# One bucket product of the attention pair loop, issued one slot earlier (slots 3 and 9 for 4 and 10)

## The chip, the cores and the metric

The kernel runs on one core of one Trainium2 chip. The metric is the device time of one execution, in microseconds (us); lower is better. Five engines of the core matter here, each with its own queue that it works through in order: TensorE (PE) for matmuls, VectorE (DVE), ScalarE (ACT) and GpSimd (POOL) for elementwise work, and SyncE (SP), which issues transfers.

## The reference

Three stages in a row. The change lies in the first, an attention over 2 x 8 heads of 768 rows and 64 features, in which a query sees only the keys that fall into its own hash bucket (six sign bits of a projection):

```python
q_bits = (np.einsum('bhsd,dk->bhsk', q, proj) > 0).astype(np.int64)
k_bits = (np.einsum('bhsd,dk->bhsk', k, proj) > 0).astype(np.int64)
q_bucket = np.sum(q_bits * powers, axis=-1)
k_bucket = np.sum(k_bits * powers, axis=-1)
mask = q_bucket[:, :, :, None] == k_bucket[:, :, None, :]
scores = scale * np.matmul(q, k.transpose(0, 1, 3, 2))
scores = np.where(mask, scores, -1000000000.0)
attn = softmax(scores)          # written out in the reference
return np.matmul(attn, v)
```

Behind it come a two-dimensional Fourier transform with normalisation and a feed-forward block (512 to 2048 to 512), and then a gated convolution with two more products.

## The kernel before, in words

The attention works on pairs of heads, eight pairs, numbered 0 to 7 (pairs 0, 1 and 7 are written out, pairs 2 to 6 are a loop; a ninth, shortened pass ends it). A pair has twelve **slots**, 0 to 11: slots 0 to 5 make the six score tiles of its head 0 (128 queries by 768 keys each), slots 6 to 11 those of its head 1. The halves 0 to 5 and 6 to 11 are called first and second half here.

In slot s TensorE makes, in this order: the scores of tile s (L1390, four matmuls into one of two score tiles in banks 0 to 3); the transposes of the probabilities of tile s-2 (L1457), three in a part called P0 and three in P1; what PREPARE lists for the slot; in slots 3 and 9 the transposes of a finished output (use "O", L1465); and in slots 2, 5, 8 and 11 twelve matmuls of probabilities times values (L1407), at the slot's end.

PREPARE is the preparation of the next head's mask. "B" projects queries and keys to bits (L1343, then VectorE's threshold L1027). "C0" and "C1" are the **bucket products**: one matmul (L1349) of the bits with a code table for the first or the second 384 columns, after which VectorE writes two comparisons, into q_b (L1031) and k_b (L1032). Those rows of q_b and k_b enter the scores of the next head, whose first tile is six slots or less away.

On the other engines a slot is: VectorE takes the row minimum of the scores (L1039), copies P1 out (L350; in slot 9 ScalarE does that, `P1_BY_ACT`), then does the comparisons of C0 or C1, or writes the output for "O" (L1056). ScalarE copies P0 out (L350) and then takes the exponential of tile s (L727). TensorE waits for the exponential of tile s-2 before the scores of tile s.

**The scratch banks.** P0, P1, B, C0, C1 and O all go to three PSUM banks (`scratch`, numbers 0 to 2), which are dealt out in turn in program order:

```python
for s in range(SLOTS):
    uses += [(s, "P0"), (s, "P1")]
    uses += [(s, task) for task in PREPARE.get(s, [])]
    if s in OUT_SLOT:
        uses.append((s, "O"))
banks = [n % 3 for n in range(len(uses))]
```

TensorE waits before each use until the use before it in the same bank has been read out (semaphores `scratch_free0` to `scratch_free2`; `wait_free`). For a bucket product the bank is free when the second comparison, k_b L1032, is done. So each use waits for the one three places ahead of it in the list (where a pair leaves a use out, as pair 0 does with O, its place is skipped, and the banks of the others stay).

Of the kernel before, what the change touches and what calls it, by code (L numbers as in the profile page):

```python
# [6 lines left out]
def attention_fft_ffn_gate_kernel(nc, qT, kT, v, proj, w_ch1, w_ch2, w_val, conv_wT, w_out,  # L7
# [20 lines left out]
    B, H, D, S = qT.shape  # L28
# [18 lines left out]
    C0 = 512  # L47
    C1 = S - C0
# [3 lines left out]
    with ctx:  # L52
# [187 lines left out]

        PREPARE = {0: ["B"], 2: ["C0"], 4: ["C1"], 6: ["B"], 8: ["C0"], 10: ["C1"]}
        C1_SLOTS = [s for s in sorted(PREPARE) if "C1" in PREPARE[s]]
        OUT_SLOT = {3: 0, 9: 1}

# [4 lines left out]
# [4 lines that stand above are left out]
# [43 lines left out]
        def wait_drained(eng, i, use):  # L298

            need(eng, scratch_free[bank_of(i, use)], use_number(i, use))  # L300
# [29 lines left out]
        def prepared(i, s, task):  # L330

            if s >= 6:
                return i, (next(x for x in range(6) if task in PREPARE.get(x, [])), task)
            if isinstance(i, int) and i == 0:
                return -1, (0, task)
            return i - 1, (next(x for x in range(6, SLOTS) if task in PREPARE.get(x, [])), task)

# [998 lines left out]
        def _(pe):  # L1336
# [10 lines left out]
            def buckets(i, use):  # L1347

                return pe.matmul(scratch(i, use), codes[:, int(use[1][1]), :], bits_sb[:, :], start=True, stop=True)  # L1349
# [5 lines left out]
            def prepare(i, use):  # L1355
# [9 lines left out]
                else:  # L1365
                    if use[1] == "C0":

                        of_head = range(6) if use[0] < 6 else range(6, SLOTS)
                        wait_drained(pe, i, (0 if isinstance(i, int) and i < 0 else
                                             next(x for x in of_head if "B" in PREPARE.get(x, [])), "B"))  # L1370
                    op = buckets(i, use)
# [430 lines left out]
```

## Time and profile before

| | before |
|---|---|
| median of 3 runs | 630.85 us (629.72 to 631.02) |
| profiled execution, its own time | 629.69 us |
| its span in the profile | 628.0 us |
| TensorE busy | 616.9 us, 98% of the span |
| VectorE, ScalarE, GpSimd busy | 55%, 51%, 40% |
| attention, pairs 0 to 7 | from 12.8 us to some 239 us of the span |

The span is the stretch between the first and the last instruction that the profiler shows; 1.7 us of the execution's own time lie around it. Busy times are averages over stages, and TensorE's ends are modelled, so that the rows below are read for their starts and for their waits.

### The profile page before, as it was taken

How to read it: one execution, taken by the hardware profiler on the slowest of the kernel's cores; microseconds unless marked ns; L12 is line 12 of the kernel's file. 1: busy time of each engine (PE TensorE's matmuls, PEld its weight loads, DVE VectorE, ACT ScalarE, POOL GpSimd, SP SyncE). 2: the span in 40 equal slices, each digit the busy share in tenths (PEclk: the TensorE clock that was granted, in tenths of full speed). 3: DMA queues.
4: the chain of work that ended last, by engine and by line, in shares of the span. 5: the costliest groups of instructions: out<-in, count | busy, mean ns of one | idle time of the engine just before them, and what ended most of it. 6: DMA issues, size and time to landing. Idle time of an engine off the chain costs nothing.

```text
span 628.0 us, 11034 instructions
## 1 busy us (share of the span) xinstructions
PE 616.9 (98%) x3754; PEld 502.4 (80%) x3754; DVE 345.9 (55%) x587; ACT 318.0 (51%) x611; POOL 250.7 (40%) x213
## 2 busy tenths in 40 slices
PE   6899999999999999999999999999999999999998
PEld 3677776777776776988888888888888888888887
DVE  3978888788888785796211111117333333339920
ACT  4877787778787783464322222225233332444242
POOL 4544433334338664356233323327444334304140
PEclk9999999999999999999999999999999999999999
DMA  6942323323332020001211222620322211000202
GB/s 142 235 112 63 89 67 85 89 75 90 96 96 70 13 64 1 1 1 34 68 60 41 68 67 67 201 68 11 90 67 67 67 57 51 10 1 1 85 18 100
DMA packets 34411, 42.15 MB, mean 67 GB/s; under 512 B 3536, under 2 KB 22480, under 8 KB 34384
## 3 DMA queue, kind: packets, MB, share of 16 engines
q1 hardware_dynamic: 32416, 37.38, 20.7%
q0 software_dynamic: 1728, 4.02, 2.7%
q10 hardware_dynamic: 240, 0.39, 0.3%
q8 instruction: 17, 0.28, 0.2%
q14 instruction: 10, 0.08, 0.0%
HBM read 38.63 MB, written 3.15 MB: 67 GB/s over the span
## 4 chain that ended last, share of the span: by engine, by line
PE 94%; DVE 2%; ACT 1%; DMA 1%; POOL 1%; issue 1%; ACTq 0%; POOLq 0%
PE banks L1608 21%; PE banks L1594 21%; PE banks L1390 12%; PE banks L1407 11%; PE banks L1457 10%; PE banks L1671 5%; PE banks L1687 5%; PE banks L1430 2%; PE banks L1540 2%; PE banks L1343 2%; PE banks L1465 1%; DMA k_raw<-in_k 1%; PE banks L1349 1%; PE banks L1514 1%; DVE row_min L1039 1%
## 5 line engine op out<-in xcount | busy, mean ns | idle before, releaser
L1170 DVE SCALAR_TENSOR_TENSOR h_lo<-banks,h_hi 128x512 fp32r<-128x512 f32 x64 | 35.3, 557 | 169.1 <-ACT h_hi L840 169.1
L1039 DVE TENSOR_REDUCE row_min<-banks 128x1 f32<-128x768 f32 x96 | 91.8, 956 | 32.2 <-PE banks L1390 31.5
L727 ACT ACTIVATE prob<-banks,row_min 128x768 f32<-128x768 f32 x96 | 87.0, 906 | 29.6 <-DVE row_min L1039 29.5
L1594 PE MATMUL banks<-unT_hi,w_hi 128*128 128x512 f32 (+1 forms) x256 | 86.2, 337 | 0.4 <-DVE h_lo L1170 0.2
L1594 PE MATMUL banks<-unT_hi,w_lo 128*128 128x512 f32 (+1 forms) x256 | 86.2, 337 | 0.0
L1594 PE MATMUL banks<-unT_lo,w_hi 128*128 128x512 f32 (+1 forms) x256 | 86.1, 336 | 0.0
L1457 PE MATMUL banks<-ident,prob 128*128 128x128 f32 x576 | 79.3, 273 | 1.4 <-ACT probT L350 1.4
L569 POOL TENSOR_TENSOR w_lo<-w_stage,w_hi 128x512 fp32r<-128x512 f32 x32 | 45.3, 1415 | 86.2 <-ACT w_hi L758 86.2
L1457 PEld LDWEIGHTS banks<-ident,prob 128*128 128x128 f32 x576 | 68.1, 140 | 6.7 <-issue 1.9
L840 ACT ACTIVATE h_hi<-banks 128x512 fp32r<-128x512 f32 x64 | 31.2, 490 | 79.0 <-PE banks L1594 79.0
L574 POOL TENSOR_TENSOR w_lo<-w_stage,w_hi 128x512 fp32r<-128x512 f32 x32 | 42.2, 1317 | 67.3 <-ACT w_hi L763 67.3
L1407 PE MATMUL banks<-probT,v_in 128*64 128x384 f32 x384 | 69.0, 494 | 0.0
L1608 PE MATMUL banks<-h_hi,w_hi 128*128 128x512 f32 (+1 forms) x256 | 66.1, 340 | 0.0
L1608 PE MATMUL banks<-h_hi,w_lo 128*128 128x512 f32 (+1 forms) x256 | 66.0, 339 | 0.0
L1608 PE MATMUL banks<-h_lo,w_hi 128*128 128x512 f32 (+1 forms) x256 | 65.6, 338 | 0.0
L763 ACT CAST w_hi<-w_stage 128x512 fp32r<-128x512 f32 x32 | 19.9, 620 | 88.8 <-PE banks L1608 88.8
L1257 DVE SCALAR_TENSOR_TENSOR x_then_u_then_gate<-x2T,taps,x_then_u_then_gate 128x384 f32<-128x384 f32 (+1 forms) x64 | 59.0, 927 | 4.9 <-DVE x_then_u_then_gate L1257 2.6
L350 ACT COPY probT<-banks 128x384 f32<-128x384 f32 x104 | 49.0, 479 | 22.5 <-PE banks L1457 22.2
L1390 PE MATMUL banks<-k_a,q_a 128*128 128x384 f32 x192 | 57.2, 378 | 2.6 <-POOL q_a L508 1.8
L503 POOL TENSOR_TENSOR k_b<-k_raw,k_a 64x768 fp32r<-64x768 f32 x16 | 29.3, 1829 | 70.2 <-ACT k_a L710 70.1
L1390 PEld LDWEIGHTS banks<-k_a,q_a 128*128 128x128 f32 x192 | 29.6, 189 | 31.4 <-issue 28.5
L1594 PEld LDWEIGHTS banks<-unT_hi,w_hi 128*128 128x128 f32 x256 | 48.0, 188 | 7.7 <-DVE h_lo L1170 0.4
(164 smaller groups left out, 1191.0 us busy)
## 6 DMA issues: line engine op xcount, KB each, us to landing
w_stage<-in_moe_w_ch SPq DMA_DIRECT2D x64, 256.0 KB, 2.8
q_raw<-in_q SPq DMA_DIRECT2D x32, 192.0 KB, 3.3
k_raw<-in_k SPq DMA_DIRECT2D x30, 192.0 KB, 3.6
v_in<-in_v SPq DMA_DIRECT2D x16, 192.0 KB, 2.8
out<-y_out SPq DMA_DIRECT2D x11, 256.0 KB, 2.0
seq_tables_sb<-in_dft POOLq DMA_DIRECT2D x6, 386.0 KB, 3.7
wvo_stage<-in_moe_w_val SPq DMA_DIRECT2D x1, 1024.0 KB, 5.7
wvo_stage<-in_moe_w_out SPq DMA_DIRECT2D x1, 1024.0 KB, 8.5
```

The lines of the kernel that those rows point to most:

```text
L350: copy(dst, src).then_inc(scratch_free[bank_of(i, use)], 1)
L569: pool.tensor_tensor(w1_lo[:, slot, :, :], w1_stage[:, slot, :, :], w1_hi[:, slot, :, :].bitcast(F32), ALU.subtract).then_inc(w1_lo_done, 1)
L574: pool.tensor_tensor(w2_lo[:, slot, :], w2_stage[:, slot, :], w2_hi[:, slot, :].bitcast(F32), ALU.subtract).then_inc(w2_lo_done, 1)
L727: act.activation(prob[s % 2][:, :, :], s_tile(s), ACT.Exp, bias=row_min[:, s:s + 1], scale=-1.0, accum_out=row_sum[:, s:s + 1]).then_inc(e ...
L1039: dve.tensor_reduce(row_min[:, s:s + 1], s_tile(s), AX.XY, ALU.min).then_inc(min_ready, 1)
L1170: dve.scalar_tensor_tensor(out=h_lo[:, slot, at:at + size], in0=h_bank[c], scalar=0.0, in1=h_hi[:, slot, at:at + size].bitcast(F32), op0=A ...
L1257: dve.scalar_tensor_tensor(out=dst, in0=src, scalar=weight, in1=dst, op0=ALU.mult, op1=ALU.add).then_inc(conv_step, 1)
L1390: op = pe.matmul(s_tile(s)[:, c, :], lhs[:, rows], rhs[:, c * HALF:(c + 1) * HALF], start=start, stop=not start)
L1407: op = pe.matmul(PS[g * D:(g + 1) * D, 7, 0:HALF], v_in[:, h, kt, :], probT[h][:, kt, g * HALF:(g + 1) * HALF], start=(kt == 0), stop=(kt ...
L1457: op = pe.transpose(bank[:, j * P:(j + 1) * P], prob[tile % 2][:, c, j * P:(j + 1) * P], ident[:, :])
L1594: op = pe.matmul(h_bank[c], w_[:, slot, kb, :], x_[:, kb, at:at + size], start=(kb == 0 and m == 0), stop=(kb == KB - 1 and m == 2))
L1608: op = pe.matmul(acc(d, c), w_[:, slot, cols], h_[:, slot, at:at + size], start=False, stop=last, skip_group_check=True)
```

## The change

The second bucket product of each head's preparation, "C1", is listed in slots 3 and 9 in place of 4 and 10. C0 and B stay where they are, and so do the outputs in slots 3 and 9. The whole diff:

```diff
-        PREPARE = {0: ["B"], 2: ["C0"], 4: ["C1"], 6: ["B"], 8: ["C0"], 10: ["C1"]}
+        PREPARE = {0: ["B"], 2: ["C0"], 3: ["C1"], 6: ["B"], 8: ["C0"], 9: ["C1"]}
         C1_SLOTS = [s for s in sorted(PREPARE) if "C1" in PREPARE[s]]
         OUT_SLOT = {3: 0, 9: 1}
```

What it moves is seen best on TensorE in slots 3 to 5 of pair 1, here before. L1465 is O, L1349 is C1, L1457 with the first wait in a slot is P0 and with the second P1; slot 3's scores stand ahead of these rows.

```order
L1457 MATMUL banks<-ident,prob1 128x128 [waits scratch_free2,exp_done]
L1457 MATMUL banks<-ident,prob1 128x128 x2
L1457 MATMUL banks<-ident,prob1 128x128 [waits scratch_free0]
L1457 MATMUL banks<-ident,prob1 128x128 x2
L1465 MATMUL banks<-ident,outT 128x128 [waits scratch_free1,outT_copied]
...
L1457 MATMUL banks<-ident,prob0 128x128 [waits scratch_free2,exp_done]
L1457 MATMUL banks<-ident,prob0 128x128 x2
L1457 MATMUL banks<-ident,prob0 128x128 [waits scratch_free0]
L1457 MATMUL banks<-ident,prob0 128x128 x2
L1349 MATMUL banks<-bits_sb,bucket_codes_sb 128x384 [waits scratch_free1]
```

The same place of the changed kernel:

```order
L1457 MATMUL banks<-ident,prob1 128x128 [waits scratch_free2,exp_done]
L1457 MATMUL banks<-ident,prob1 128x128 x2
L1457 MATMUL banks<-ident,prob1 128x128 [waits scratch_free0]
L1457 MATMUL banks<-ident,prob1 128x128 x2
L1349 MATMUL banks<-bits_sb,bucket_codes_sb 128x384 [waits scratch_free1]
L1465 MATMUL banks<-ident,outT 128x128 [waits scratch_free2,outT_copied]
...
L1457 MATMUL banks<-ident,prob0 128x128 [waits scratch_free0,exp_done]
L1457 MATMUL banks<-ident,prob0 128x128 x2
L1457 MATMUL banks<-ident,prob0 128x128 [waits scratch_free1]
L1457 MATMUL banks<-ident,prob0 128x128 x2
```

C1 now takes bank 1 in slot 3, ahead of O, O takes bank 2, which P0 of slot 3 had, and in slot 4 P0 goes from bank 2 to bank 0 and P1 from bank 0 to bank 1, which C1 had three uses earlier.

On VectorE the two comparisons of C1 moved up with it. Slots 3 to 5 of pair 1, before (L1039 is the row minimum, L350 the copy of P1, L1056 the output):

```order
L1039 TENSOR_REDUCE row_min<-banks 128x1 [waits scores_done]
L350 COPY probT0<-banks 128x3x128 [waits scratch_full0]
L1056 TENSOR_TENSOR x_then_u_then_gate<-banks,row_inv 128x3x2x64 [waits inv_step,scratch_full1]
L1039 TENSOR_REDUCE row_min<-banks 128x1 [waits scores_done]
L350 COPY probT0<-banks 128x3x128 [waits scratch_full0]
L1031 TENSOR_SCALAR q_b1<-banks,bucket_ones_sb 64x384 [waits scratch_full1]
L1032 TENSOR_SCALAR k_b1<-banks,bucket_ones_sb 64x384
L1039 TENSOR_REDUCE row_min<-banks 128x1 [waits scores_done]
```

And in the changed kernel:

```order
L1039 TENSOR_REDUCE row_min<-banks 128x1 [waits scores_done]
L350 COPY probT0<-banks 128x3x128 [waits scratch_full0]
L1031 TENSOR_SCALAR q_b1<-banks,bucket_ones_sb 64x384 [waits scratch_full1]
L1032 TENSOR_SCALAR k_b1<-banks,bucket_ones_sb 64x384
L1056 TENSOR_TENSOR x_then_u_then_gate<-banks,row_inv 128x3x2x64 [waits inv_step,scratch_full2]
L1039 TENSOR_REDUCE row_min<-banks 128x1 [waits scores_done]
L350 COPY probT0<-banks 128x3x128 [waits scratch_full1]
L1039 TENSOR_REDUCE row_min<-banks 128x1 [waits scores_done]
```

Both comparisons stand ahead of the output and of slot 4's row minimum now; before they stood behind them. The number of instructions is the same on both engines.

## Rows read from the trace of the kernel before

**Rows 1.** The page's first part: busy us, share of the span, instructions.

```profile
PE 616.9 (98%) x3754; PEld 502.4 (80%) x3754; DVE 345.9 (55%) x587; ACT 318.0 (51%) x611; POOL 250.7 (40%) x213
```

**Rows 2.** Windows of the trace: busy us by engine, then granted clock, DMA share.

```profile
10.00:30.00 20.00, 16.37 (x105) 12.10 (x105) 17.07 (x26) 14.92 (x30) 12.55 (x14) 1.00 0.70 185
30.00:228.00 198.00, 198.00 (x1330) 142.54 (x1326) 165.38 (x268) 153.35 (x311) 88.25 (x62) 1.00 0.29 78
```

**Rows 3.** Waits of TensorE up to 250 us: total us, times, longest.

```profile
PE banks L1457 <- ACT probT L350: 1.4, 2, 1.1
...
PE banks L1390 <- DVE k_b L1032: 0.3, 1, 0.3
```

**Rows 4.** The chain that ended last, pieces in slots 9 to 11, pairs 0 and 3.

```profile
34.70 0.96 PE banks L1390 x4
...
119.53 0.33 PE banks L1465 x3
...
121.21 0.17 PE banks L1349
121.39 0.71 PE banks L1390 x4
```

**Rows 5.** Timeline, slots 3 to 5 of pair 7: start us, us, instruction.

```profile
219.70 0.82 PE L1457 MATMUL banks<-ident,prob 128*128 128x128 f32 x6
219.90 0.96 DVE L1039 TENSOR_REDUCE row_min<-banks 128x1 f32<-128x768 f32 x1 [0.68 <-PE banks L1390]
220.22 0.48 ACT L350 COPY probT<-banks 128x384 f32<-128x384 f32 x1 [0.57 <-PE banks L1457]
...
220.77 0.55 DVE L350 COPY probT<-banks 128x384 f32<-128x384 f32 x1
...
221.40 0.82 PE L1457 MATMUL banks<-ident,prob 128*128 128x128 f32 x6
...
222.56 0.55 DVE L350 COPY probT<-banks 128x384 f32<-128x384 f32 x1
...
222.93 0.83 PE L1457 MATMUL banks<-ident,prob 128*128 128x128 f32 x6
223.15 0.61 DVE L1031 TENSOR_SCALAR q_b<-banks,bucket_ones_sb 64x384 fp32r<-64x384 f32 x1
...
223.77 0.62 DVE L1032 TENSOR_SCALAR k_b<-banks,bucket_ones_sb 64x384 fp32r<-64x384 f32 x1
```

**Rows 6.** Timeline, slots 9 to 11 of pair 3, in the loop.

```profile
118.72 0.82 PE L1457 MATMUL banks<-ident,prob 128*128 128x128 f32 x6
118.92 0.96 DVE L1039 TENSOR_REDUCE row_min<-banks 128x1 f32<-128x768 f32 x1 [0.68 <-PE banks L1390]
119.24 0.86 ACT L350 COPY probT<-banks 128x384 f32<-128x384 f32 x2 [0.49 <-PE banks L1457]
...
119.37 0.49 PE L1465 MATMUL banks<-ident,outT 128*128 128x128 f32 x3
...
120.17 0.56 DVE L1056 TENSOR_TENSOR x_then_u_then_gate<-banks,row_inv 128x384 f32 x1 [0.30 <-PE banks L1465]
...
120.40 0.82 PE L1457 MATMUL banks<-ident,prob 128*128 128x128 f32 x6
...
120.97 0.42 PE L1349 MATMUL banks<-bits_sb,bucket_codes_sb 128*128 128x384 f32 x1
```

**Rows 7.** Timeline, slots 3 to 6 of pair 0.

```profile
20.34 0.47 ACT L350 COPY probT<-banks 128x384 f32<-128x384 f32 x1
20.47 0.55 DVE L350 COPY probT<-banks 128x384 f32<-128x384 f32 x1
...
20.95 0.85 PE L1457 MATMUL banks<-ident,prob 128*128 128x128 f32 x6 [1.07 <-ACT probT L350]
...
23.05 0.62 DVE L1032 TENSOR_SCALAR k_b<-banks,bucket_ones_sb 64x384 fp32r<-64x384 f32 x1
...
23.73 0.62 PE L1390 MATMUL banks<-k_a,q_a 128*128 128x384 f32 x2 [0.34 <-DVE k_b L1032]
```

## The prediction

> **What bounds the kernel now.** I read the page first: TensorE is busy for 98% of the span, the others for half of it or less [rows 1]. A share over the whole program says little about one place, so the windows of the trace come next: between 30 and 228 us, that is from pair 0's second half to slot 7 of pair 7, TensorE is busy for 198.00 of 198.00 us, VectorE for 165.38 and ScalarE for 153.35 [rows 2]. Then the waits: up to 250 us TensorE waits for a copy of a scratch bank twice, 1.4 us in all, and for the comparison k_b once, 0.3 us [rows 3], and both of the waits that matter here lie in pair 0 [rows 7]. So the reader is to see an engine that never waits in the steady attention. The chain that ended last runs there from one piece of TensorE to the next [rows 4]. It follows that nothing is to be gained there by an earlier bucket product: nobody waits for it. A half pair takes its time because TensorE's queue is full, and any new wait on TensorE is paid in full, unless an older wait behind it gives it back. The work behind the attention hangs on its results, so a later end moves the rest by as much.
>
> **What the change adds: a wait at P1 of slot 4 (and 10).** TensorE's instructions are the same, in another order. C1 is one matmul of 0.17 us in the chain [rows 4]; it is taken from slot 4 and put into slot 3, so by itself it is 0. VectorE's two comparisons move too: 0.61 and 0.62 us [rows 5]. What is new is who has the scratch bank that P1 of slot 4 takes. Before, it was P1 of slot 3, read out by one copy. Now it is C1 of slot 3, which is free only when both comparisons are done, and they stand behind slot 3's row minimum and copy on VectorE.
>
> *First halves (slots 3 to 5), by starts, from [rows 5].* VectorE: the row minimum of slot 3 starts at 219.90 and the copy of P1 at 220.77. From a copy to the first comparison it is 223.15 - 222.56 = 0.59 us, and from there to the end of the second 223.77 + 0.62 - 223.15 = 1.24. So C1's bank is free at 220.77 + 0.59 + 1.24 = 222.60. TensorE: the transposes of slot 4 start at 221.40; with C1 in front they start 0.17 later, at 221.57, and P1, their second half, 0.33 later (half of a group that takes some 0.66 of the engine), at 221.90. How long from the free bank to the restart? Two rows of pair 0 bound it [rows 7]: comparison k_b ends at 23.67 and the scores start at 23.73, 0.06; ScalarE's copy ends at 20.81 and the transposes start at 20.95, 0.14. I take 0.10. P1 of slot 4 then starts at 222.70, **0.80 us late**. What stands behind it on TensorE is P1, slot 5 and its product with the values: the whole half. Nothing gives it back: scores of slot 5 need an exponential that does not move, and VectorE's and ScalarE's lag is worked off during the product with the values, as it is now. Slot 4's row minimum comes about 1.3 us later than now (the two comparisons stand ahead of it), and its exponential with it, but TensorE asks for that one only in slot 6, four or more us on. The new wait of O (bank 2, ScalarE's copy of P0, ended at 220.22 + 0.48 = 220.70) costs 0.3 us at most and lies ahead of the same restart: it is covered. Seven first halves have all this (pairs 1 to 7): 7 x 0.80 = 5.6 us.
>
> *Second halves (slots 9 to 11), from [rows 6].* P1 of slot 9 is copied by ScalarE, so VectorE is free for C1 at 118.92 + 0.87 = 119.79. C1's matmul would start where O follows the transposes now less what a transposed weight takes longer: a bucket product starts 120.97 - 120.40 = 0.57 after its transposes, so at 118.72 + 0.57 = 119.29, and it ends at 119.71. VectorE starts on it 0.04 to 0.30 later (0.30 is what O shows in this loop); I take 0.18, 119.89. The comparisons end 1.24 later, 121.13, and P1 restarts at 121.23. Unhindered it would start at 120.40 + 0.17 + 0.33 = 120.90: **0.33 late**. O gives nearly the same: its bank is free when ScalarE has copied P0, 119.24 + 0.48 = 119.72, so it starts at 119.82 in place of 119.37 + 0.17 = 119.54, 0.28 late. The two overlap, and the larger counts. Six halves (pairs 1 to 6): 6 x 0.33 = 2.0 us.
>
> *Pair 0 and the end.* In pair 0 the first half has no O. C1's bank is free at 20.47 + 0.58 + 1.24 = 22.29, P1 restarts at 22.39, where it now starts at 20.95 + 0.33 = 21.28; C1 is out of slot 4 (-0.17), and the wait of 0.34 for the same comparison at 23.73 goes [rows 7]. 1.11 - 0.17 - 0.34 = 0.6; I take 0.5, since the restart may fall into the shadow of ScalarE. In its second half O's 0.33 is missing in front of P1, so the wait is 0.33 + 0.33 = 0.66, and the scores of slot 11, which take 0.96 there for 0.71 elsewhere [rows 4], give 0.25 back: 0.4. In pair 7 no C1 is made in slot 9, but O still takes P0's bank and waits for ScalarE: 0.3.
>
> **The sum.** 5.6 + 2.0 + 0.5 + 0.4 + 0.3 = 8.8 us. The profiled execution took 629.69 us, which gives 638.5; it is at the lower end of the runs, whose median is 630.85, which would give 639.65. A median of new runs may fall at either level, so I take 639.0.
>
> **Starts or pieces.** The sum goes by TensorE's starts. The chain's pieces, laid end to end, give less: there P1 of a first half is reached 0.17 us later (a start lies that much ahead of the modelled end before it) and the price is 0.63, and a second half costs 0.19. That is 7 x 0.63 + 6 x 0.19 + 1.2 = 6.7 us, 636.4 to 637.6. The Trainium skill, page Perfetto Trace Analysis, section "Summary: the profiler window per engine type", says that on TensorE the start is observed and the end an estimate; by that the starts are the better ruler, and the sum would be 8.8 and not 6.7. The rows cannot decide it, so both are in the range.
>
> **Rivals.**
> - *The wait is partly given back* (2 to 5 us in all, 632 to 635.5). For it: VectorE is idle for 0.68 us ahead of slot 3's row minimum [rows 5], so it does catch up. Against it: TensorE is the engine that has no slack, and its own queue is in order. 0.15.
> - *No change, the reason for waiting is not there.* C1's bank would have to be free when P1 comes, that is VectorE 0.70 us earlier in slot 3 (222.60 against 221.90). Its row minimum hangs on the scores of the same slot [rows 5], so nothing lets it start earlier. 630 to 631. 0.05.
> - *Faster.* In pair 0 TensorE waits 1.07 us for ScalarE's copy of P0 and 0.34 us for k_b [rows 7]. The change takes both reasons away: P0 of slot 4 now needs bank 0, copied by VectorE, and C1 is ready earlier. If P1's wait were nil, 1.41 us would go: 629.4 on the median's level, 628.3 on the profiled one's. It decides at the same point as above, and in pair 0 the row minimum and copy of slot 3 are themselves late (the copy starts at 20.47), so 1.07 stays nearly whole even so. 0.04.
> - *Much slower.* Waits inside the loop may cost more than these, since there registers are worked out between the matmuls: 0.3 us (the gap that O shows) at each of 15 places is 4.5 more, 643.5. 0.04. The granted clock is 1.00 also between 10 and 30 us, where TensorE is idle for 3.63 of 20 us and once for 1.07 in a row [rows 2, 7]; the new idle time is 0.3 to 0.8 at a time. A fall to the lower level would double the column time after each wait: for one slot of 1.36 us after 15 waits that is 20 us, 659. The Trainium skill, page TensorE: Matmul & The Clock Gate, section "A second HAM failure mode: psum-queue depth-cycling", tells of a clock that goes up and down when a kernel cycles through PSUM banks and TensorE idles briefly in each round; that would be this case, and no row here shows it. 0.01.
>
> **How the numbers follow.** The forecast (waits of 0.2 to 0.9 at the places named, 635.5 to 642) has 0.71, and with the rivals 0.15, 0.05, 0.04 and 0.05 that makes 1. The range reaches from 634.5, where all waits cost the pieces' price less a part that is given back, to 642, which is the sum on the median's level with 0.15 more for each of 15 waits. It leaves out some 0.2. A measurement of this kernel tells changes from about 0.2% (1.3 us). Slower by more than that: forecast, partial return and much slower, 0.91; within it 0.05; faster 0.04.
>
> **What would show it.** In the changed profile TensorE should be idle ahead of L1457, released by VectorE's k_b L1032, once in every half pair: about 0.8 us before P1 of slot 4, 0.3 before P1 of slot 10. The list of waits should name "PE banks L1457 <- DVE k_b L1032" with 12 or more times and 6 to 8 us in all, and O (L1465) waiting for ScalarE's probT. A pair should take 1.1 us more than now; the second half of the program should be as long as now and merely start later. VectorE's busy time stays at 345.9. The prediction is wrong if the waits are there but the pairs are not longer (something else bound them), if C1's comparisons finish before TensorE reaches P1, or if waits appear at the scores for an exponential (slot 4's, now 1.3 us later), which I hold to be hidden.

## The result, and the profile after

| | before | changed |
|---|---|---|
| median | 630.82 us (629.72 to 631.02, 4 runs) | 639.61 us (639.43 to 640.53, 4 runs) |
| profiled execution, its span | 629.69, 628.0 | 640.53, 638.8 |

The ratio of the times is 1.0146, with a 95% interval of 1.0128 to 1.0164: **slower by 1.5%, 8.8 us between the medians**. The prediction was 639.0, with a range of 634.5 to 642.0.

The first lines of the page of the changed kernel (busy us, share of the span, instructions):

```profile
span 638.8 us, 11044 instructions
...
PE 623.7 (98%) x3754; PEld 503.3 (79%) x3754; DVE 344.7 (54%) x587; ACT 317.8 (50%) x611; POOL 250.8 (39%) x213
```

TensorE's share still reads 98%, as in [rows 1]: a share is blind to a wait that the modelled ends of the matmuls fill. (The instructions are the same 3754, yet their busy time reads 6.8 us more.) The chain that ended last is not. In pairs 3 and 4 of the changed kernel it leaves TensorE in both halves (start us, us, what; the four starts of B, L1343, mark the halves):

```profile
117.66 0.78 PE banks L1343 x8
...
124.51 0.34 PE banks L1457 x3
124.85 0.02 issue
124.88 0.49 ACT probT L350
125.36 0.14 issue
125.50 0.52 PE banks L1465 x3
...
132.39 0.78 PE banks L1343 x8
...
139.30 0.71 DVE row_min L1039
...
140.18 0.54 DVE probT L350
...
141.38 0.63 DVE k_b L1032
142.01 0.04 issue
142.06 0.55 PE banks L1457 x3
...
147.60 0.78 PE banks L1343 x8
...
162.34 0.78 PE banks L1343 x8
```

Between 132.39 and 147.60 lies a first half: 15.21 us. The engine that sets its end is VectorE in slot 3 (row minimum, copy, both comparisons), and TensorE goes on at P1 of slot 4, 0.05 us after the end of k_b. Between 117.66 and 132.39, and again to 162.34, lies a second half: 14.73 and 14.74 us. There the chain goes over ScalarE's copy of P0 and resumes at O.

The timeline of slots 3 and 4 of that first half, to be laid beside [rows 5]:

```profile
138.29 0.62 PE L1390 MATMUL banks<-k_a,q_a 128*128 128x384 f32 x2
...
139.10 0.82 PE L1457 MATMUL banks<-ident,prob 128*128 128x128 f32 x6
139.30 0.96 DVE L1039 TENSOR_REDUCE row_min<-banks 128x1 f32<-128x768 f32 x1 [0.68 <-PE banks L1390]
...
140.17 0.55 DVE L350 COPY probT<-banks 128x384 f32<-128x384 f32 x1
...
140.75 0.61 DVE L1031 TENSOR_SCALAR q_b<-banks,bucket_ones_sb 64x384 fp32r<-64x384 f32 x1
...
141.25 0.49 PE L1457 MATMUL banks<-ident,prob 128*128 128x128 f32 x3
141.38 0.62 DVE L1032 TENSOR_SCALAR k_b<-banks,bucket_ones_sb 64x384 fp32r<-64x384 f32 x1
...
142.06 0.55 PE L1457 MATMUL banks<-ident,prob 128*128 128x128 f32 x3 [0.32 <-DVE k_b L1032]
...
142.50 0.95 DVE L1039 TENSOR_REDUCE row_min<-banks 128x1 f32<-128x768 f32 x1
```

P0 starts at 141.25 and P1 at 142.06. Three transposes take 0.33 us when nothing holds them, so P1 is 142.06 - 141.25 - 0.33 = 0.48 us late against P0. P0 itself is 0.28 us late, since O ahead of it was held up by ScalarE's copy: from the start of slot 3's transposes to that of slot 4's it was 221.40 - 219.70 = 1.70 us in [rows 5], and with C1's 0.17 that makes 1.87; here it is 141.25 - 139.10 = 2.15. Together that is 0.76. The idle time in brackets is only 0.32. The total of the waits understates the price for the same reason (TensorE up to 260 us of the changed kernel: total us, times, longest; the third row is that of the weight loads):

```profile
PE banks L1457 <- DVE k_b L1032: 3.3, 9, 0.7
...
PE banks L1465 <- ACT probT L350: 1.6, 9, 0.3
...
PEld banks L1457 <- DVE k_b L1032: 5.4, 9, 0.9
```

**Where the 10.8 us between the two profiled spans lie**, by the starts of B in both timelines. Up to slot 0 of pair 0 the changed kernel is 1.2 us late (14.92 against 13.70) before it has done anything in another order. Pair 0: 1.2 and 0.1; some 0.5 of the 1.2 goes with the lower clock told of below, as the same order at the full clock takes 0.7 (kernel with slots 3 and 10). First halves: 0.86 in pair 1, 0.73 in each of pairs 2 to 6, 0.80 in pair 7, 5.3 in all. Second halves: 0.34 in pair 1 and 0.37 in each of pairs 2 to 6, 2.2 in all. Pair 7's second half: 0.4. The whole rest of the program, some 389 us: 0.3.

Pair 0 has its own mechanism. No product with the values stands in its slot 5, so nothing covers the late row minimum of slot 4: the chain goes from k_b to that row minimum (24.06) and the exponential (to 26.05), and the scores of slot 6 wait for it.

```profile
24.06 0.97 DVE row_min L1039
...
25.05 1.00 ACT prob L727 x2
...
26.19 0.95 PE banks L1390 x4
```

The first 1.2 us are not the change's. In the windows of the changed kernel (busy us of PE, PEld, DVE, ACT and POOL, then the granted clock) TensorE runs there at half of its clock:

```profile
10.00:13.00 3.00, 2.69 (x6) 1.00 (x4) 2.47 (x4) 2.44 (x4) 2.86 (x2) 0.56 0.27 80
13.00:17.00 4.00, 3.63 (x14) 1.99 (x15) 1.46 (x2) 0.98 (x2) 2.04 (x2) 0.50 0.16 39
...
40.97:220.67 179.70, 176.38 (x1165) 124.06 (x1165) 144.02 (x234) 133.19 (x270) 75.47 (x50) 1.00 0.29 77
```

A clock of 0.50 is the lower level, 1.2 GHz. Ahead of it TensorE had stood idle for 0.96 us for the first bits; the first transfer of keys had landed at 8.39 us, against 7.86 in the profile of before. It is not a matter of the new order: of the twelve profiled executions here six have such a stretch of 3 to 7 us, each once, between 9 and 27 us of the span, and one of the six is the kernel before with slot 3's P1 by ScalarE. All four runs of the changed kernel have a mean clock of 0.994 to 0.997, as runs with such a stretch do. The kernel before has 45 runs beside these experiments: with a mean clock of 1.000 their median is 630.16 us (27 runs), with 0.997 it is 630.91 (16 runs), so a comparison of single profiles, and of medians too, carries some 0.7 us of this. The three other runs of the changed kernel had spans of 637.8 to 638.0 us; against the kernel before the change is worth 9 to 10 us of span. With the waits, between 41 and 221 us, the clock is 1.00.

### The profile page after: what moved, and what is told of

Its sections match the earlier page's. It is cut to its first block, busy times and chain, and to the rows that moved or that the text cites. A ratio compares the mean times of both kernels' runs of the same rounds, so it can differ in the third digit from the quotient of the medians.

```text
span 638.8 us, 11044 instructions
## 1 busy us (share of the span) xinstructions
PE 623.7 (98%) x3754; PEld 503.3 (79%) x3754; DVE 344.7 (54%) x587; ACT 317.8 (50%) x611; POOL 250.8 (39%) x213
## 4 chain that ended last, share of the span: by engine, by line
PE 90%; DVE 5%; ACT 1%; issue 1%; DMA 1%; POOL 1%; ACTq 0%; DVEq 0%; POOLq 0%
PE banks L1608 21%; PE banks L1594 20%; PE banks L1390 11%; PE banks L1407 10%; PE banks L1457 8%; PE banks L1671 5%; PE banks L1687 5%; PE banks L1430 2%; PE banks L1540 2%; PE banks L1343 2%; DVE row_min L1039 2%; DVE k_b L1032 1%; DMA k_raw<-in_k 1%; PE banks L1514 1%; DVE probT L350 1%
## 5 line engine op out<-in xcount | busy, mean ns | idle before, releaser
L1039 DVE TENSOR_REDUCE row_min<-banks 128x1 f32<-128x768 f32 x96 | 91.6, 955 | 43.6 <-PE banks L1390 43.3
L1457 PE MATMUL banks<-ident,prob 128*128 128x128 f32 x576 | 80.9, 274 | 4.0 <-DVE k_b L1032 3.3
L1457 PEld LDWEIGHTS banks<-ident,prob 128*128 128x128 f32 x576 | 68.0, 140 | 11.1 <-DVE k_b L1032 5.4
L350 ACT COPY probT<-banks 128x384 f32<-128x384 f32 x104 | 49.0, 479 | 39.5 <-PE banks L1457 39.4
L1390 PE MATMUL banks<-k_a,q_a 128*128 128x384 f32 x192 | 58.7, 387 | 1.4 <-ACT prob L727 0.7
```

The lines of the kernel that those rows point to most:

```text
L350: copy(dst, src).then_inc(scratch_free[bank_of(i, use)], 1)
L1039: dve.tensor_reduce(row_min[:, s:s + 1], s_tile(s), AX.XY, ALU.min).then_inc(min_ready, 1)
L1390: op = pe.matmul(s_tile(s)[:, c, :], lhs[:, rows], rhs[:, c * HALF:(c + 1) * HALF], start=start, stop=not start)
L1457: op = pe.transpose(bank[:, j * P:(j + 1) * P], prob[tile % 2][:, c, j * P:(j + 1) * P], ident[:, :])
```

## The experiments

All kernels were compared with the kernel before on the same chip, where its median was 630.07 to 630.40 us; the ratio is therefore the measure, and "us over before" is worked out from it. The last two columns are the lengths of a half pair in the loop, from the start of B to the start of the next B in the profile; from one pair of the loop to the next they differ by up to 0.06.

| kernel | median us | ratio to before (95%) | first half | second half |
|---|---|---|---|---|
| before | 630.82 | | 14.50 | 14.35 |
| changed | 639.61 | 1.0146 (1.0128 to 1.0164) | 15.21 | 14.74 |
| C1 in slots 3, 10 | 635.68 | 1.0084 (1.0070 to 1.0098) | 15.18 | 14.40 |
| C1 in slots 4, 9 | 633.22 | 1.0048 (1.0034 to 1.0061) | 14.50 | 14.70 |
| changed, O ahead of C1 | 634.82 | 1.0068 (1.0054 to 1.0082) | 14.74 | 14.57 |
| changed, slot 3's P1 by ScalarE | 635.25 | 1.0079 (1.0065 to 1.0093) | 14.76 | 14.73 |
| changed, slot 9's P1 by VectorE | 641.81 | 1.0181 (1.0167 to 1.0195) | 15.20 | 15.20 |
| changed, one comparison more | 647.24 | 1.0264 (1.0248 to 1.0280) | 15.73 | 15.27 |
| before, one comparison more | 630.66 | 1.0004 (0.9995 to 1.0013) | 14.50 | 14.36 |
| before, slot 3's P1 by ScalarE | 630.52 | 1.0003 (0.9994 to 1.0012) | 14.48 | 14.35 |
| before, slot 9's P1 by VectorE | 630.51 | 1.0001 (0.9992 to 1.0010) | 14.50 | 14.36 |
| C1 in slots 5, 11 | 635.29 | 1.0085 (1.0071 to 1.0100) | 14.81 | 14.66 |

**Only the first halves.** (The edits of the experiments are shown against the changed kernel, where nothing else is said.)

```diff
-        PREPARE = {0: ["B"], 2: ["C0"], 3: ["C1"], 6: ["B"], 8: ["C0"], 9: ["C1"]}
+        PREPARE = {0: ["B"], 2: ["C0"], 3: ["C1"], 6: ["B"], 8: ["C0"], 10: ["C1"]}
```

> C1 in slots 3 and 10, so only the first halves have the new order. Theory of the bank wait: P1 of slot 4 waits about 0.8 us for comparison k_b in seven halves, 5.6, and 0.5 in pair 0: 6.1 us over the kernel before, about 637.0. Rival (the two halves share one cause further on, such as a later exponential, and do not add): anything else, above all the whole 8.8 or nothing.

Measured: 635.68 us, 0.84% or 5.3 us over before; the theory had 6.1, and the steps between the starts of B make 5.6, since pair 0's second half gets 0.3 back. The chain of this kernel in pair 3:

```profile
99.71 0.78 PE banks L1343 x8
...
108.67 0.64 DVE k_b L1032
...
109.35 0.55 PE banks L1457 x3
...
114.89 0.78 PE banks L1343 x8
```

The half takes 15.18 us, as in the changed kernel, and its end is set by k_b.

**Only the second halves.**

```diff
-        PREPARE = {0: ["B"], 2: ["C0"], 3: ["C1"], 6: ["B"], 8: ["C0"], 9: ["C1"]}
+        PREPARE = {0: ["B"], 2: ["C0"], 4: ["C1"], 6: ["B"], 8: ["C0"], 9: ["C1"]}
```

> C1 in slots 4 and 9, only the second halves have the new order. Theory of the bank wait: 6 x 0.33 = 2.0, 0.4 in pair 0, 0.3 in pair 7: 2.7 us over the kernel before, about 633.5; its first halves without any wait of TensorE. Rival as for the first halves alone: 8.8 or nothing.

Measured: 633.22 us, 0.48% or 3.0 us over before; the theory had 2.7. Its first halves are as before, 14.50. The two parts add up within the noise: 5.3 + 3.0 = 8.3 against 9.2 for both by the ratio (1.46%); the intervals are about 0.9 us wide to either side, for both together 1.1. But the chain does not name k_b:

```profile
113.49 0.78 PE banks L1343 x8
...
120.69 0.49 ACT probT L350
121.18 0.05 issue
121.22 0.55 PE banks L1465 x3
...
128.19 0.78 PE banks L1343 x8
```

It goes over ScalarE's copy of P0, whose bank O takes now.

**O ahead of C1.** The list of the scratch uses is made in the other order, so that the same tiles get other neighbours in the banks.

```diff
             uses += [(s, "P0"), (s, "P1")]
-            uses += [(s, task) for task in PREPARE.get(s, [])]
             if s in OUT_SLOT:
                 uses.append((s, "O"))
+            uses += [(s, task) for task in PREPARE.get(s, [])]
```

> C1 stays in slots 3 and 9, but O is issued ahead of it, so that P1 of slot 4 follows O in its bank and P0 of slot 5 follows C1. VectorE's work is the same and slot 4's row minimum is as late as in the changed kernel. Theory of the bank wait: O is read out at 221.79 on the scale of the first half in the trace of before, so P1 of slot 4 does not wait; P0 of slot 5 waits some 0.2 us for C1, and in second halves C1 itself waits 0.2 for ScalarE's copy: 13 x 0.2 plus 0.5 is 3 us, about 633.5, and the wait for k_b stands at slot 5. Rival (the cost is the late row minimum and exponential of slot 4, not the bank): as slow as the changed kernel, 639.6.

Measured: 634.82 us. In the loop it decides against the late row minimum. The timeline of this kernel, slots 3 and 4 of pair 3:

```profile
106.55 0.62 PE L1390 MATMUL banks<-k_a,q_a 128*128 128x384 f32 x2
...
109.39 0.82 PE L1457 MATMUL banks<-ident,prob 128*128 128x128 f32 x6
...
110.88 0.96 DVE L1039 TENSOR_REDUCE row_min<-banks 128x1 f32<-128x768 f32 x1
```

Slot 4's row minimum starts 110.88 - 106.55 = 4.33 us after slot 3's scores, where the changed kernel has 142.50 - 138.29 = 4.21: it is even later, and the half takes 14.74 us in place of 15.21. P0 and P1 of slot 4 run as one group of 0.82, with no gap. What remained (0.2 a half) is C1's own wait for ScalarE's copy of P0 (the chain gives C1 0.35 us in place of 0.17), and in first halves P0 of slot 5, which starts 0.06 us after the end of k_b (110.85), as expected. The theory had 633.5; what it missed lies in pair 0, whose first half takes 13.63 us for 11.58. There C1 waits 1.6 us for that copy, since ScalarE is behind at this point, and slot 6's scores wait 0.75 us for the late exponential of slot 4: in pair 0 the rival does cost time. The granted clock was 0.50 from 14.4 to 17.6 us of this profile as well; the parts were not separated.

```profile
22.13 0.44 PE L1349 MATMUL banks<-bits_sb,bucket_codes_sb 128*128 128x384 f32 x1 [1.60 <-ACT probT L350]
...
26.02 0.59 PE L1390 MATMUL banks<-k_a,q_a 128*128 128x384 f32 x2 [0.75 <-ACT prob L727]
```

**P1 of slot 3 by ScalarE**, which lets VectorE start on C1 earlier; and the same edit in the kernel before, as a control.

```diff
-        P1_BY_ACT = (9,)
+        P1_BY_ACT = (3, 9)
```

> The changed kernel with P1 of slot 3 copied by ScalarE too, as it is in slot 9, so that VectorE starts on C1 right after slot 3's row minimum (0.58 us earlier). Theory of the bank wait: a first half costs what a second does, 0.3 in place of 0.8, so 7 x 0.5 = 3.5 us less than the changed kernel, about 636; k_b is still what TensorE waits for. Rival (VectorE is simply overloaded in the half, or ScalarE is near its limit too): no gain, 639 or more. The same copy moved in the kernel before left its time as it was (630.52 against 630.4).

> Control: the kernel before with P1 of slot 3 copied by ScalarE. TensorE does not wait for VectorE there, so the theory gives no change, 630.0 to 631.0 (at most the 0.1 us waits of slot 5 in the loop go, 0.5 us); if ScalarE were near its limit it would be slower.

Measured: 635.25 us, 4.4 less than the changed kernel (theory: 3.5). By the starts, from pair 0 to the end, it is 3.3. The rest fits the clock: four of the five runs have a mean clock of 1.000, none of the changed kernel's has. First halves take 14.76 and are now like second ones, 14.73. In the kernel before the edit changes nothing (ratio 1.0003). That k_b would still be what TensorE waits for was wrong: the chain goes over ScalarE's copy and O in both halves. Here a first half:

```profile
107.87 0.49 ACT probT L350
108.36 0.04 issue
108.41 0.55 PE banks L1465 x3
```

**P1 of slot 9 by VectorE**, the opposite, with its control.

```diff
-        P1_BY_ACT = (9,)
+        P1_BY_ACT = ()
```

> The changed kernel with P1 of slot 9 copied by VectorE, so that a second half has the instructions of a first. In the changed kernel second halves wait for ScalarE's copy of P0 (at O) and not for k_b. Theory: with the copy ahead of C1's comparisons k_b ends some 0.57 us later and becomes what TensorE waits for at P1 of slot 10, so a second half takes 15.2 us in place of 14.74: 6 x 0.47 plus some 0.5 in pair 0, 3 to 3.5 us more than the changed kernel, 642.6 to 643.1. Rival (the second halves' cost is ScalarE's copy alone, VectorE has room): no change or a gain, since ScalarE has one copy less, 639 or less.

> Control: the kernel before with P1 of slot 9 copied by VectorE. There the first halves show what a second half would then be: about 14.5 us in place of 14.35, so 0 to 1 us more than before, 630.4 to 631.4. If VectorE's load as such were the cost in the run beside it, this one would be slower by as much, 3 us.

Measured: 641.81 us, 2.2 more than the changed kernel and below the 642.6 to 643.1 that were expected. All halves take 15.18 to 15.20 us: 0.46 more in each second half, as expected, seven times 3.2 with pair 0's. From pair 7 on the profile is 0.5 us shorter than that of the changed kernel, for which no run gives a reason. And four of the five runs have a mean clock of 1.000, while the changed kernel's have 0.997 or less, so that its median is the higher for it. That accounts for the missing 1 us within the noise. The list of waits names k_b 15 times:

```profile
PE banks L1457 <- DVE k_b L1032: 5.0, 15, 0.7
```

The control stands at 1.0001, where a load of VectorE as such would have cost 3 us.

**One comparison more on C1's bank**, between the two that are there, written to a spare tile (not in the prologue). In the kernel before and in the changed one:

```diff
                     dve.tensor_scalar(q_b[h][low, cols], src[top, :], code_ones[top, :], None, ALU.is_equal)
+                    if c == 1 and not (isinstance(i, int) and i < 0):
+                        dve.tensor_scalar(spare[low, :], src[top, :], code_ones[top, :], None, ALU.is_equal)
```

> The kernel before, with one more comparison of C1's bank on VectorE, 0.61 us, written to a spare tile, so that C1's bank is free 0.62 us later in each half (not in the prologue). Theory: in slots 4 and 10 nobody waits for C1's bank and VectorE catches up during the product with the values, so 0 to 1 us more than before, 630.8 to 631.8. Rival (VectorE's work in a half counts, wherever it lies): 15 x 0.62 = 9.3 us more, 640.

> The changed kernel with the same extra comparison. Theory of the bank wait: every 0.62 us that C1's bank is held longer is paid in full at P1 of slots 4 and 10, 13 x 0.62 = 8.1 and some 1.1 in pair 0: 9 us more than the changed kernel, about 648.5. Rival (part of the wait is given back, or the price is something other than the time the bank is held): well under 9 us more, 640 to 644.

Measured: in the kernel before 630.66 us, ratio 1.0004, nothing beyond the noise, though VectorE has 15 instructions and 7.9 us of busy time more (353.8 for 345.9). Its halves are as long as before, but for the first of pair 0, 12.09 for 11.58, where the scores of slot 6 waited 0.34 us for k_b [rows 7] and now wait 0.9. In the changed kernel 647.24 us, 7.6 more. The timeline of the latter, slot 3 of pair 3, shows the size of the addition:

```profile
113.60 0.61 DVE L1032 TENSOR_SCALAR q_b<-banks,bucket_ones_sb 64x384 fp32r<-64x384 f32 x1
...
114.14 0.60 DVE L1034 TENSOR_SCALAR spare<-banks,bucket_ones_sb 64x384 fp32r<-64x384 f32 x1
...
114.75 0.62 DVE L1035 TENSOR_SCALAR k_b<-banks,bucket_ones_sb 64x384 fp32r<-64x384 f32 x1
...
115.43 0.55 PE L1460 MATMUL banks<-ident,prob 128*128 128x128 f32 x3 [0.84 <-DVE k_b L1035]
```

(Lines are three further down in this kernel.) From q_b to k_b it is 1.15 us in place of 0.63 in the changed kernel (140.75 to 141.38), so the bank is held 0.52 us longer and not 0.62, and first halves are longer by just that: 15.73 for 15.21. 13 halves by 0.53 are 6.9. Pair 0 has 1.6 more, and the sum of 8.5 is above the 7.6 between the medians; the five runs lie 2.8 us apart, 645.76 to 648.58. In pair 0 a second effect comes in. TensorE waits 1.20 us in a row for k_b there, and behind this wait the granted clock falls to the lower level for some 3.8 us (from 20 to 23 us and from 27 to 30 it is 1.00; this is the window between):

```profile
23.00:27.00 4.00, 3.75 (x17) 3.65 (x18) 3.00 (x5) 1.74 (x4) 3.52 (x9) 0.57 0.67 186
```

The same order without the added comparison takes 12.26 us for this half at the full clock (kernel with slots 3 and 10), here it is 13.83: 0.5 for the bank, and some 1.0, by subtraction, with the lower clock. Second halves grow by 0.53 too, and now they wait for k_b. Since the whole 0.52 comes out there too, k_b must have been level with O's wait within a few hundredths of a microsecond.

**The other way, slots 5 and 11.** Shown against the kernel before:

```diff
-        PREPARE = {0: ["B"], 2: ["C0"], 4: ["C1"], 6: ["B"], 8: ["C0"], 10: ["C1"]}
+        PREPARE = {0: ["B"], 2: ["C0"], 5: ["C1"], 6: ["B"], 8: ["C0"], 11: ["C1"]}
```

> C1 moved the other way, to slots 5 and 11. Theory: P1 of slot 4 and both parts of slot 5 have banks that were copied out long ago, so no bank wait; but C1's comparisons then end after the product with the values has begun, at about the time the next head's scores want them, 0.1 to 0.3 us late in each of 15 halves: 2 to 4 us more than before, 632.5 to 635, with TensorE's scores L1390 waiting for k_b. Rival (a bucket product's place costs only where it displaces a bank): the same as before, 630.8.

Measured: 635.29 us, 0.85% over before; a half pair in the loop is 0.3 us longer, and the next head's scores wait for k_b:

```profile
112.68 0.62 DVE L1032 TENSOR_SCALAR k_b<-banks,bucket_ones_sb 64x384 fp32r<-64x384 f32 x1
...
113.64 0.61 PE L1390 MATMUL banks<-k_a,q_a 128*128 128x384 f32 x2 [0.30 <-DVE k_b L1032]
```

This k_b ends at 112.68 + 0.62 = 113.30, within 0.04 us of where TensorE would have started the scores (113.34, the end of the product with the values in the chain); yet they start at 113.64, 0.34 after k_b, and in the second half behind it again 0.34 after (127.96 to 128.30). In pair 1, which is written out, they start 0.11 after k_b (54.53 to 54.64), and the half is only 0.08 longer. So the comparisons are hardly late, and it is going on behind this wait inside the loop that costs 0.3; what takes the time there is not shown. The steady part was sized rightly (13 x 0.3 = 3.9 at most), by luck in part, since the expectation had a late k_b for it. Pair 0 was not: 13.37 us for 11.58 in its first half, since no product with the values stands there to cover the comparisons. Of the five placings tried, slots 4 and 10 have the fewest waits; no kernel here beats the one before.

## Why the prediction was right, point by point

- *What bounds the kernel.* Right in the loop. VectorE's work can be moved or added to in the kernel before without a measurable effect (three controls within 0.04%, with intervals of 0.09% to either side), and in the changed kernel every such edit shows on TensorE.
- *First halves, P1 of slot 4 waits for k_b, 7 x 0.80 = 5.6.* Right in place, cause and size: 5.3. In the two written-out pairs a half is 0.86 and 0.80 longer. In the loop it is 0.73: the loop's first halves were 14.50 long before, against 14.35 in pair 1, and the new wait seems to swallow the 0.15. What the 0.15 is stays open; it is there as well with P1 of slot 3 copied by ScalarE and with one comparison more. O's wait (0.28) and P1's (0.48) lie one behind the other in pair 4, and k_b sets their sum: O's is covered, as written. The restart comes 0.05 us after k_b (142.01 to 142.06), where I took 0.10.
- *Second halves, 6 x 0.33 = 2.0.* Right in size, 2.2, wrong in the step "the larger counts": I put C1's comparisons at 0.33 and O's wait for ScalarE at 0.28. It is O's wait that binds; it restarts 0.14 us after the copy ends (125.36 to 125.50), and k_b is just under it. Both are waits for a bank that the rotation handed on, so the sum did not suffer, but "k_b once in every half pair" was wrong: it is named nine times, O nine times.
- *Pair 0, 0.5 + 0.4, and 0.3 in pair 7.* Near in size, incomplete in mechanism. I held slot 4's late exponential to be hidden everywhere; in pair 0 slot 6's scores wait 0.2 us for it (at 26.19 in the changed kernel). The first half alone costs 0.7 in pair 0 (12.26 against 11.58 in the kernel with slots 3 and 10), the second alone 0.4 (15.05 against 14.61 in the one with 4 and 9). Together the second one adds only 0.1, as the late first half takes a wait out of it (14.28 with slots 3 and 10). 0.8 in all against 0.9. Pair 7: 0.4 against 0.3.
- *The sum 8.8 and the two levels.* The medians differ by 8.8. By the steps it is 5.3 + 2.2 + 0.8 + 0.4 = 8.7. That the sum fits to 0.1 is luck: the terms are off by -0.3, +0.2, -0.1 and +0.1, and the interval of the ratio reaches from 8.1 to 10.3 us. The two levels overlap (629.67 to 631.04 at a mean clock of 1.000, 629.76 to 631.74 at 0.997), so the stretch at the lower clock is at most a part of what sets them apart. A pair of the loop takes 1.1 us more, as was written.
- *Starts or pieces.* The starts were the right ruler: 6.7 by the pieces was too little. The Trainium skill (page Perfetto Trace Analysis, section "Summary: the profiler window per engine type") has the end of a TensorE instruction as an estimate; the trace agrees, for it shows 0.32 us of idle time in a half that is 0.73 longer. That also explains my one wrong picture of the profile, "idle about 0.8 us before P1". The list of waits has 3.3 us where I expected 6 to 8, and the waits of the weight loads, 5.4 us, come nearer.
- *Rivals.* Nothing was given back in the loop, and there the late exponential cost nothing, as the run with O ahead of C1 shows; in pair 0 it cost time. A fall of the clock by the new waits did not come in the loop: 1.00 over 180 us with a wait in every half. With one comparison more, though, the clock fell in pair 0 behind a wait of 1.20 us. Inside the loop P1 goes on 0.05 us after k_b, so there the waits cost no more than elsewhere; at the next head's scores they do, as slots 5 and 11 show.

## What to carry to other kernels

Where a few buffers are dealt out in turn, an operation's place in the list decides not only when it runs but whose release everything behind it waits for. Ask of each move which use now stands as many places behind it as there are buffers, and when the reader of the moved one ends. A tile that takes two instructions and a queue to read out wants a place where its buffer is not asked for again soon and its results are not yet wanted. Of the places tried here that is slot 4: in slot 3 the bank is asked for too early, in slot 5 the bank is free in time but the next head's scores want the results. The price can be worked out from the starts of one profile, to a tenth of a microsecond per round; the idle times in brackets can't be used for it on TensorE.

## What was not expected of the hardware

- TensorE's restart after a wait took 0.04 to 0.06 us when VectorE released it, and either 0.14 (at 125.36 of the changed kernel) or 0.04 to 0.05 (121.18 with slots 4 and 9, 108.36 with slot 3's P1 by ScalarE) when ScalarE did. What tells the two apart was not tried. At the scores of the next head inside the loop it took 0.34 behind VectorE's k_b, with slots 5 and 11.
- An added comparison of 0.60 us cost VectorE 0.52 us from start to start, between two others that read the same bank.
- The granted clock fell to 0.50 for 3 to 7 us, once, in six of twelve profiled executions, always between 9 and 27 us. The longest time in a row that TensorE had stood idle shortly before was 0.96 us in the changed kernel, 1.20 with one comparison more and 1.78 with O ahead of C1; yet the kernel before stood idle for 1.78 us (until 12.84), and the one with slots 5 and 11 for 2.02 (until 25.77), with the clock at 1.00 throughout. So the length of one idle stretch does not tell, and what does was not tried.
